# Chunked attention before two dense layers: a first tile with paced loads, and probabilities turned by VectorE in the loop

## The reference

```python
# attention: batch 4, 8 heads, 768 positions, head width 64; chunks of 32 queries
# each chunk sees 8 memory keys and its own 32 keys with 16 to the left and 8 to the right (64 keys, edges masked)
scores = scale * (q_c @ k_full.T); scores -= scores.max(-1)
a = exp(scores); a = a / (a.sum(-1) + 1e-9)
out[:, :, c_start:c_end] = a @ v_full
x = out.transpose(0, 2, 1, 3).reshape(3072, 512)
h = x @ w_in;  x = max(0.01 * h, h) @ w_out              # 512 -> 2048 -> 512, first layer
h = x @ w_in2; P = a0 + a1*h + a2*h^2 + a3*h^3           # second layer
Q = 1 + |b0|*|h| + |b1|*h^2; y = (P / (Q + 1e-6)) @ w_out2
```

## Time and profile before

| | |
|---|---|
| runs, us | 1151.1, 1153.5, 1154.75; median 1153.5 |
| profiled execution: time, us | 1152.93 |
| profiled execution: span, us | 1151.1 |
| granted TensorE clock, mean | 0.997 |
| TensorE matmul busy | 1136.9 us, 99% |
| VectorE busy | 741.6 us, 64% |
| ScalarE busy | 565.9 us, 49% |
| GpSimd busy | 132.6 us, 12% |

### The profile page before, as it was taken

One profiled execution on the slowest core, in us unless ns is written; L12 is line 12 of the kernel. 1 busy time (PEld: TensorE's weight loads), 2 busy tenths in 40 slices (PEclk: granted clock), 3 DMA queues, 4 the chain that ended last, 5 costly groups with the idle time before them and its releaser, 6 DMA issues.

```text
span 1151.1 us, 22841 instructions
## 1 busy us (share of the span) xinstructions
PE 1136.9 (99%) x8950; PEld 1066.0 (93%) x8950; DVE 741.6 (64%) x1385; ACT 565.9 (49%) x1184; POOL 132.6 (12%) x132
## 2 busy tenths in 40 slices
PE   7999999999999999999999999999999999999998
PEld 6999999999999999999999999999999999999996
DVE  5554444444445454443327888888888888888886
ACT  4223223323233332322227676676767667676765
POOL 4991120211202112100000000000000000000000
PEclk8999999999999999999999999999999999999999
DMA  7662434334434255210786010020201002020000
GB/s 265 198 201 102 169 108 156 130 114 157 163 131 154 74 184 175 83 56 2 285 278 241 1 65 18 1 83 1 83 1 71 13 1 83 1 83 1 28 1 28
DMA packets 44311, 114.77 MB, mean 100 GB/s; under 512 B 5040, under 2 KB 5168, under 8 KB 44208
## 3 DMA queue, kind: packets, MB, share of 16 engines
q1 hardware_dynamic: 44208, 113.33, 28.5%
HBM read 77.66 MB, written 35.65 MB: 98 GB/s over the span
## 4 chain that ended last, share of the span: by engine, by line
PE 95%; DVE 2%; ACT 1%; issue 1%; DMA 0%; SPq 0%; DVEq 0%
PE psum L512 15%; PE psum L514 15%; PE psum L513 15%; PE psum L527 8%; PE psum L546 8%; PE psum L547 8%; PE psum L545 8%; PE psum L528 7%; PE psum L529 7%; PE psum L484 2%; PE psum L461 1%; PE psum L469 1%; DVE g_lo L860 1%; DVE scratch L857 0%; ACT g_hi L688 0%
## 5 line engine op out<-in xcount | busy, mean ns | idle before, releaser
L512 PE MATMUL psum<-x_hi,w_hi 128*128 128x384 f32 x1020 | 342.5, 336 | 1.5 <-DVE x_lo L851 1.5
L514 PE MATMUL psum<-x_hi,w_lo 128*128 128x384 f32 x1020 | 342.6, 336 | 0.0
L513 PE MATMUL psum<-x_lo,w_hi 128*128 128x384 f32 x1020 | 341.6, 335 | 0.0
L857 DVE TENSOR_TENSOR scratch<-psum,scratch 128x384 f32<-128x384 f32 x128 | 71.3, 557 | 237.6 <-ACT scratch L682 236.9
L682 ACT ACTIVATE scratch<-psum 128x384 f32<-128x384 f32 x128 | 62.8, 491 | 279.2 <-PE psum L514 275.3
L512 PEld LDWEIGHTS psum<-x_hi,w_hi 128*128 128x128 f32 x1020 | 191.5, 188 | 8.4 <-issue 2.3
L513 PEld LDWEIGHTS psum<-x_lo,w_hi 128*128 128x128 f32 x1020 | 191.5, 188 | 5.4
L514 PEld LDWEIGHTS psum<-x_hi,w_lo 128*128 128x128 f32 x1020 | 191.4, 188 | 0.0
L527 PE MATMUL psum<-g_hi,w_hi 128*128 128x384 f32 x512 | 177.5, 347 | 0.0
L529 PE MATMUL psum<-g_hi,w_lo 128*128 128x384 f32 x512 | 171.3, 335 | 0.0
L528 PE MATMUL psum<-g_lo,w_hi 128*128 128x384 f32 x512 | 171.2, 334 | 0.0
(11 more groups left out here) (75 smaller groups left out, 1407.4 us busy)
## 6 DMA issues: line engine op xcount, KB each, us to landing
raw<-weights_in SPq DMA_DIRECT2D x64, 256.0 KB, 4.1
scratch<-groups_in SPq DMA_DIRECT2D x21, 768.0 KB, 6.1
scratch<-groups_in SPq DMA_DIRECT2D x21, 512.0 KB, 4.4
w_hi_scratch<-w_high SPq DMA_DIRECT2D x32, 256.0 KB, 4.1
w_lo_scratch<-raw SPq DMA_DIRECT2D x32, 256.0 KB, 4.5
w_hi<-w_hi_scratch SPq DMA_DIRECT2D x32, 256.0 KB, 3.6
w_lo<-w_lo_scratch SPq DMA_DIRECT2D x32, 256.0 KB, 4.5
x_hi_scratch<-x_hi SPq DMA_DIRECT2D x8, 768.0 KB, 3.3
```

Source lines behind the costliest of these rows:

```text
L512: nc.tensor.matmul(bank, hi, x_hi[:, b, k, :], start=(k == 0), stop=False)
L513: nc.tensor.matmul(bank, hi, x_lo[:, b, k, :], start=False, stop=False)
L514: last = nc.tensor.matmul(bank, lo, x_hi[:, b, k, :], start=False, stop=(k == KT - 1))
```

## The change

In the loop each group of attention takes three places instead of four: scores at f, `TURN_AT` at f + 1, values at f + 3, with the rounding of the heads in that same step.

- VectorE makes the maximum and one 8-wide product with -scale (`loop_maxima`); the subtraction of 512 columns is gone.
- ScalarE makes eight exponentials of 64 columns with row sums (`loop_exp`) in place of one of 512.
- VectorE (`turn_probs`) adds the small number, inverts (8 wide), multiplies the 512 columns of probabilities in SBUF, and turns them with eight block transposes, each of 32 partitions by 256 columns. VectorE's row sum, TensorE's four transposes and ScalarE's copy are gone.
- TensorE's values wait for `probs_turned`; scores wait for `turned` and no more for `x_ready`. The small matmuls are as many and as large as before, in another order and with another placing of heads in the arrays.
- VectorE turns the heads straight out of PSUM (`turn_values`); the division there is gone.

In the first tile the order on VectorE and ScalarE changes: group 1 now has VectorE's subtraction and row sum and ScalarE's one exponential, as group 0 had; only group 2 keeps eight exponentials. The heads are rounded and subtracted after all three groups are through. The loads have a semaphore each, and SyncE issues transfer n after transfer n-4 has landed; the first weight slice is issued ahead of the last two value transfers. `keep_warm(13)` is 12, and 34 small matmuls on zeros follow.

```diff
-TRANSPOSE_AT = {f + 1: g for f, g in SCORES_AT.items()}
-VALUES_AT = {f + 2: g for f, g in SCORES_AT.items()}
-SAVE_AT = {f + 3: g for f, g in SCORES_AT.items()}
+TURN_AT = {f + 1: g for f, g in SCORES_AT.items()}
+VALUES_AT = {f + 3: g for f, g in SCORES_AT.items()}
...
+            for n, (c, at) in enumerate(PIECES):
+                if n >= 4:
+                    sp.wait_ge(first_loaded[n - 4], 16)
+                sp.dma_start(grp[c][:, at:at + 512], groups[c, :, at:at + 512]).then_inc(first_loaded[n], 16)
+                if n == GPT * QK_PIECES - 1:
+                    sp.dma_start(ident[:, :], ident_in).then_inc(ident_loaded, 16)
+                if n == len(PIECES) - V_PIECES - 1:
+                    load_raw(0, 0, first=True)
...
             def wait_scores(g, c, own_place=False):
-                pe.wait_ge(qk_loaded[ring(c)], loads(g, c, (Q_W + K_W) // 512))
-                if not own_place:
-                    pe.wait_ge(x_ready, g)
+                if own_place:
+                    for n in range(QK_PIECES):
+                        pe.wait_ge(first_loaded[QK_PIECES * g + n], 16)
+                else:
+                    pe.wait_ge(qk_loaded[ring(c)], loads(g, c))
+                    pe.wait_ge(turned, g)
...
             def values(c, at):
+                for cc in range(CPG):
+                    for j in range(SLOTS):
+                        for st in range(SETS):
+                            q0 = (j % 2) * 2 * P + (j // 2 * CPG + cc) * CHUNK
+                            last = nc.tensor.matmul(
+                                at.loop_values_at[CHUNK * j:CHUNK * (j + 1), st, :, cc, :],
+                                at.probs_t[DH * st:DH * (st + 1), q0:q0 + CHUNK],
+                                v_of(ring(c), st, j, cc), start=True, stop=True)
+                last.then_inc(heads_ready, 1)
...
-                        if f in TRANSPOSE_AT:
-                            transpose_probs(g0 + TRANSPOSE_AT[f], loop_att[TRANSPOSE_AT[f]])
...
-            keep_warm(13)
+            keep_warm(12)
+            keep_warm_small(34)
...
+            def loop_exp(g, at):
+                act.wait_ge(shifted, g + 1)
+                for u in range(2):
+                    for c in range(CPG):
+                        n = CPG * u + c
+                        last = nc.scalar.activation(at.loop_probs[:, n, :], at.scores[:, u, c, :], ACT.Exp,
+                                                    scale=SCALE, bias=at.safe[:, n:n + 1],
+                                                    accum_out=at.loop_sums[:, n:n + 1])
+                last.then_inc(exp_ready, 1)
...
             exp_scores(0, first_att[0])
-            first_exp(1, first_att[1])
+            exp_scores(1, first_att[1])
             save_probs_t(0, first_att[0])
             save_probs_t(1, first_att[1])
             first_exp(2, first_att[2])
-            save_heads(0, 0, 0, first_att[0])
             save_probs_t(2, first_att[2])
-            save_heads(1, 1, 0, first_att[1])
-            save_heads(2, 2, 0, first_att[2])
+            save_first_heads(0, 0, 0, first_att[0])
+            save_first_heads(1, 1, 0, first_att[1])
+            save_first_heads(2, 2, 0, first_att[2])
...
+            def turn_probs(g, at):
+                dve.wait_ge(exp_ready, g + 1)
+                nc.vector.tensor_scalar(at.safe, at.loop_sums, SUM_EPS, None, ALU.add).then_inc(sums_ready, 2)
+                dve.wait_ge(sums_ready, 3 * g + 2)
+                nc.vector.reciprocal(at.loop_inv, at.safe).then_inc(sums_ready, 1)
+                dve.wait_ge(sums_ready, 3 * g + 3)
+                nc.vector.tensor_tensor(at.loop_probs, at.loop_probs,
+                                        at.loop_inv.unsqueeze(2).broadcast_to([P, SETS * CPG, KEYS]),
+                                        ALU.mult).then_inc(normalised, 1)
+                dve.wait_ge(normalised, g + 1)
+                for q in range(SLOTS):
+                    for h in range(2):
+                        to = CHUNK * (q // 2 * 2 + h)
+                        last = nc.vector.transpose(
+                            at.probs_t[to:to + CHUNK, (q % 2) * 2 * P:(q % 2 + 1) * 2 * P].rearrange("p (n k) -> p n k", k=CHUNK),
+                            at.loop_halves[CHUNK * q:CHUNK * (q + 1), :, h, :])
+                last.then_inc(probs_turned, 1)
+
+            def turn_values(g, at):
+                dve.wait_ge(heads_ready, g + 1)
+                nc.vector.transpose(at.probs_t.rearrange("p (s n) -> p s n", s=SETS), at.loop_values).then_inc(turned, 1)
...
             shift_scores(0, 0, 0, 0, first_att[0])
-            first_maxima(1, first_att[1])
+            shift_scores(1, 1, 0, 0, first_att[1])
             sum_rows(0, first_att[0])
             first_maxima(2, first_att[2])
-            first_inverses(1, first_att[1])
+            sum_rows(1, first_att[1])
             normalise(0, first_att[0])
             turn_heads(0, first_att[0])
             normalise(1, first_att[1])
             turn_heads(1, first_att[1])
             first_inverses(2, first_att[2])
-            save_heads_low(0, 0, 0, first_att[0])
             normalise(2, first_att[2])
             turn_heads(2, first_att[2])
+            save_heads_low(0, 0, 0, first_att[0])
             save_heads_low(1, 1, 0, first_att[1])
             save_heads_low(2, 2, 0, first_att[2])
```

More of the change, by code:

```diff
@@ L136, in build @@
     S = nc.alloc_semaphore
-    qk_loaded = [S(f"qk_loaded{j}") for j in range(3)]
-    v_loaded = [S(f"v_loaded{j}") for j in range(3)]
+    qk_loaded = [S(f"qk_loaded{j}") for j in range(2)]
+    v_loaded = [S(f"v_loaded{j}") for j in range(2)]
     raw_loaded = [S(f"raw_loaded{j}") for j in range(RAW)]
+    first_loaded = [S(f"first_loaded{n}") for n in range(GPT * GRP_W // 512)]
     ident_loaded = S("ident_loaded")
@@ L161, in build @@
     probs_t_ready = S("probs_t_ready")
+    probs_turned = S("probs_turned")
     heads_ready = S("heads_ready")
@@ L245, in ring, with loads @@
         return c if c < 3 else c % 2
[L247 to L251, removed]
+    def loads(g, c):
+        return (g - c % 2) * 8 + (0 if c % 2 else -16)
+    PIECES = [(c, at) for lo, hi in ((0, Q_W + K_W), (Q_W + K_W, GRP_W)) for c in range(GPT) for at in range(lo, hi, 512)]
+    QK_PIECES, V_PIECES = (Q_W + K_W) // 512, V_W // 512
     with nc.Block() as block:
@@ L320, in _ @@
             sp.sem_inc(y_stored, 1)
[L323 to L333, removed]
+            for n, (c, at) in enumerate(PIECES):
[6 more added lines that the diff above has]
+                    load_raw(0, 0, first=True)
+            for j in range(1, RAW):
+                sp.wait_ge(first_loaded[len(PIECES) - 4 + j], 16)
                 load_raw(j, j, first=True)
@@ L493, in keep_warm, with keep_warm_small @@
                     nc.tensor.matmul(psum[:, H_BANKS[1], 0:TILE], g_hi[:, 0, 0:P], g_hi[:, 0, :], start=True, stop=True)
+            def keep_warm_small(count):
+                zeros = g_hi[:, 0, :].bitcast(F32)
+                for n in range(count):
+                    r0, j = DH * (n % 2), n // 2 % SLOTS
+                    nc.tensor.matmul(psum[CHUNK * j:CHUNK * (j + 1), H_BANKS[n % 2], 0:KEYS], zeros[r0:r0 + DH, 0:CHUNK],
+                                     zeros[r0:r0 + DH, 0:KEYS], start=True, stop=True)
             def wait_weights(f, half, second):
@@ L613, in first_scores @@
                 wait_scores(g, g, own_place=True)
-                scores(g, first_att[g])
+                scores_first(g, first_att[g])
             def first_values(g):
-                wait_values(g, g)
-                values(g, first_att[g])
+                wait_values(g, g, own_place=True)
+                values_first(g, first_att[g])
             pe.wait_ge(zeros_ready, 1)
-            keep_warm(13)
+            keep_warm(12)
+            keep_warm_small(34)
             first_scores(0)
@@ L813, in first_maxima, with loop_maxima, save_low @@
                 nc.vector.tensor_scalar(at.safe, at.st[:, 0, :], -SCALE, None, ALU.mult).then_inc(shifted, 1)
+            def loop_maxima(g, gi, tp, t, at):
+                dve.wait_ge(scores_ready, g + 1)
+                edge = None
+                if tp == 0 and gi == 0:
+                    edge = at.scores[:, :, 0, N_MEM:N_MEM + LEFT]
+                if tp == 1 and gi == GPT - 1:
+                    edge = at.scores[:, :, CPG - 1, KEYS - RIGHT:KEYS]
+                if edge is not None:
+                    nc.vector.tensor_scalar(edge, edge, NEG, None, ALU.add).then_inc(masked, 1)
+                    dve.wait_ge(masked, t + 1)
+                first_maxima(g, at)
+            def turn_probs(g, at):
[8 more added lines that the diff above has]
+                dve.wait_ge(normalised, g + 1)
+                for q in range(SLOTS):
+                    for h in range(2):
[7 more added lines that the diff above has]
```

(6 more changed lines are left out.)

73 lines of the change are left out of this document (49 added, 24 removed).

## The result

The changed kernel takes 1160.2 us (median of 4 runs, 1158.7 to 1162.6), the kernel before 1153.4 (4 runs, 1151.1 to 1154.75): ratio 1.0066, 95% interval 1.0051 to 1.0080. It is slower by 6.8 us by the medians and 7.6 by the ratio; 1143.7 was forecast.

What follows compares the result with a forecast made beforehand. The loop was taken as bound by what TensorE issues: -12.1 us shed there, +3.0 of new waits, -0.7 in the first tile, -9.8 in all, giving 1143.7 us. The forecast holds between 1138.5 and 1148.

Steps and rivals of the forecast that it cites:

- both waits of the earlier trace: Loop, TensorE: 1.5 us for `x_lo` ahead of scores and 0.9 us for the exponential ahead of transposes would go.
- the waits for the turn: Loop: TensorE's new waits for VectorE's turned probabilities, 3.0 us in all (from 0 to 6.5).
- the 8-wide product takes the 0.17 of the like instruction: Loop, VectorE after the maximum: the product with -scale takes 0.17 us, so it is done at 149.0.
- 0.4 to 0.8 us of margin: Loop: turned probabilities ready 0.4 us before TensorE asks, 0.8 where GpSimd's work doesn't lengthen the step's low part.
- rival B: Loop: GpSimd holds the multiplication and low parts in most groups, 0.3 to 0.7 us a group; 1150; chance 0.06.
- so rarely: Loop: GpSimd works 125 of 596 us, mostly in the first tile, so it would seldom hold VectorE.
- the 1.3 allowed: Loop beyond its first three groups: 0.1 us of waiting a group on average over 18 groups, taken as 1.3 us.
- The short transposes: Loop, VectorE: eight transposes of 32 partitions by 256 columns, 0.37 us apart, 3.0 us for eight.
- rival A: Loop: the turn is late in every group, as each transpose keeps its 0.64 us; 1179; chance 0.10.
- The first tile: Start of the kernel: new order and loads gain 0.7 us, from 0.3 up to 3 if the clock stays up.
- A load per 0.7 us: First tile: with four loads under way one lands every 0.7 us, as the queue does now; pacing costed at 0.
- rival C: First tile: four loads under way starve it; landings of 4.1 us, a load per 1.0 us; 1146; chance 0.06.

Runs made afterwards that it cites:

- small_off_lock: Changed kernel with the loop's maxima put into PSUM and the 8-wide addition of 1e-9 to the row sums left out; 1145.9 us, ratio 0.9950.
- unpaced: Changed kernel without the wait for transfer n-4 and without the waits ahead of the weights; 1160.4 us, ratio 1.0071.
- loop_only: Changed kernel with the old first tile (loads queued at once, old order, 13 warm-up matmuls); 1155.7 us, ratio 1.0037.

## Why the prediction was wrong

**Right.** TensorE bounds the loop; transposes at 0.46 a group came off; both waits of the earlier trace rows went; scores and values kept their price; with the holds gone, the waits for the turn are 3.3 us (`small_off_lock`) where 3.0 was forecast; in the rest of the loop a group without stalls is as forecast (501.7 against 512.07 once the stalls are gone, 10.4 us over 18 groups). Phase B stood still.

**The step that failed** is "the 8-wide product takes the 0.17 of the like instruction". That was read from one row in the quiet second tile. The trace of before held a warning: VectorE's group of L828 from 24 to 100 us, the same 8-wide form, has a mean of 421 ns:

```profile
L828 DVE TENSOR_SCALAR stats<-stats 128x8 f32<-128x8 f32 x3 | 1.3, 421 | 0.1
```

Two of these three took 0.54 and 0.55. It cost nothing there, as the inverse was wanted only two steps later. The change put two such instructions on the one path that had been given 0.4 to 0.8 us of margin, and each took up to 1.1 us more. In the first two groups both were held, in the third the product alone. I weighed GpSimd's hold only for the multiplication, which measured 0.692 in the median and 0.836 at most. So rival B named the holder and, in the main, the wrong instructions. Its price of 0.3 us a group was too low in the fifteen steps, where GpSimd is at work for 49.4 of the 51.4 us up to 85.5: 11.9 us in three groups. Beyond those "so rarely" failed: 9 of 18 products were held, and the stalls are 5 us against the 1.3 allowed. The same section of the Trainium skill that I cited ("SBUF — State Buffer", Who interferes with whom) also says that `tensor_scalar` can take the shared port pair, while `tensor_reduce` doesn't; the runs agree (beside GpSimd the product takes 0.37 to 1.25 from SBUF and 0.166 to 0.167 from PSUM, the maximum L880 at most 0.69), and show that 8 columns don't spare it.

**Mis-sized.** The short transposes stand 0.45 apart and not 0.37. The chain of the changed kernel in its last group, without GpSimd: 

```profile
530.09 0.17 DVE L900 TENSOR_SCALAR stats<-stats 128x8 f32<-128x8 f32 x1
530.29 0.20 DVE L902 RECIPROCAL stats<-stats 128x8 f32<-128x8 f32 x1
530.53 0.69 DVE L904 TENSOR_TENSOR scratch<-scratch,stats 128x512 f32<-128x512 f32 x1
531.25 3.58 DVE L911 STREAM_TRANSPOSE scratch<-scratch 32x256 f32<-32x256 f32 x8
```

4.74 us from start to end, where 0.5 + 0.7 + 3.1 = 4.3 was taken. This ate most of the margin without a stall of its own (rival A didn't come: groups without GpSimd have none). A term that was missing altogether is the clock in the loop: two stretches of 3.41 us at 0.50, after pauses of 3.63 and 3.11, worth up to 3.4 of the 11.9 us. `small_off_lock`, whose longest wait is 1.8 us, has no such stretch. The 0.24 us behind each wait was missing too. No kernel had the waits without the fall of the clock, so its price is read from the granted clock and not from a run of its own.

**The first tile** was forecast at -0.7 and measured +1.7 us in front of the old loop, +2.4 in front of the quiet one. "A load per 0.7 us" is a wrong step: with four under way each landing took 4.1, as rival C had it, so a load per 1.0 us and the third scores 1.5 later, at 11.40. Group 2's transposes started at 17.64 where 15.1 was forecast. How much of the time this costs stays open, as the split above is not settled. The low parts behind the last turn cost somewhat more than was said (1.04, 1.09 and 1.76 us, 3.7 in all instead of 3.1). Rival C's chance of 0.06 was too low: the row of 4.1 had been in front of me and I took the first load's 2.8.

## What to carry to other kernels

Before a chain is put on a path with less than a microsecond to spare, look up every instruction of it, the shortest too, in the stretch where the other engines are busiest, and take its longest duration there, not one row from elsewhere. Even that may be too low: 0.55 us was the longest here before the change, 1.25 after it. The safer price is the length of the instruction that can hold it, 1.3 us here; an 8-wide instruction took nearly all of it. Don't price such holds by the other engine's busy share: at 12% it met half of the products. Give the short instruction another source, drop it, or cut the holder's instructions. Moving a consumer later didn't help here, since the engine that follows it works in order and stood waiting.

## What the hardware showed that was not expected

- A `tensor_scalar` of 8 columns from SBUF to SBUF took up to 1.25 us beside GpSimd and ended 0.03 us after GpSimd's instruction; from PSUM it took 0.166 to 0.167. Block transposes in SBUF (0.432 to 0.444) were not held, 16 of 168 having started beside GpSimd. The reciprocals of 8 columns took 0.202 to 0.205, but only two of 21 met an instruction of GpSimd and none met its subtraction, so little can be said of them.
- A block transpose of 32 partitions by 256 columns takes 0.435 us, and eight in a row stand 0.45 apart.
- Four transfers of 256 KB under way gave 276 GB/s where an unbounded queue gave 389.
- In the small matmuls of the first tile TensorE stopped for 0.4 to 2.2 us with nothing shown to wait for: 1.15 in the kernel before, 1.07 and 2.21 in `unpaced`, 0.44 and 0.71 in the changed kernel, none over 0.3 in `loop_only`. Why was not tested.
